# Attention and two FFN blocks on one core: the values product in high and low parts

## What is computed

```python
# attention: q, k, v are (4, 8, 576, 64), s is (4, 8, 576)
scores = scale * np.matmul(q, k.transpose(0, 1, 3, 2))
cum = np.cumsum(np.maximum(s, 0.0), axis=-1)
bias = -(cum[:, :, :, None] - cum[:, :, None, :])
scores = np.where(causal, -1000000000.0, scores + np.minimum(bias, 0.0))
attn = np.exp(scores - np.max(scores, axis=-1, keepdims=True))
attn = attn / (np.sum(attn, axis=-1, keepdims=True) + 1e-09)
x = np.matmul(attn, v)                    # heads side by side: (4, 576, 512)
# first FFN: x @ w_in (512 x 1024), relu h, 3-tap convolution c along the sequence,
x = (h * sigmoid(c)) @ w_out              # 1024 x 512
# second FFN: low-rank mixing along the sequence, then
u = x + (x^T @ U @ V)^T
out = u + relu(u @ w_ch1) @ w_ch2         # 512 x 2048, 2048 x 512
```

## Time and profile before

| | us |
|---|---|
| median of 3 runs | 1060.52 (1055.34 to 1065.8) |
| profiled execution, its own time | 1059.91 |
| its span, first to last instruction | 1058.1 |
| busy: PE / DVE / ACT / POOL | 947.3 / 506.0 / 348.7 / 170.4 |

### The profile page before, as it was taken

The page is one execution under the profiler, slowest core; times in us unless marked ns, Lnnn a source line. Parts: engine busy times, 40 slices in busy tenths (PEclk is TensorE's granted clock), DMA queues, the critical chain, the costliest instruction groups (busy, mean ns, idle before and its releaser), DMA issues.

```text
span 1058.1 us, 16893 instructions
## 1 busy us (share of the span) xinstructions
PE 947.3 (90%) x6395; PEld 881.2 (83%) x6395; DVE 506.0 (48%) x735; ACT 348.7 (33%) x662; POOL 170.4 (16%) x110
## 2 busy tenths in 40 slices
PE   3888887979999997988999999897999999789998
PEld 2766777869999987977899898796989999669998
DVE  4478884474344367165425247447334437332121
ACT  2445453443335144243323215334322314232020
POOL 2222164311333023000000003201000003100000
PEclk9899998998999999987999989899899999889999
DMA  4575554635665753342444544343255374223441
GB/s 96 137 206 159 132 152 146 210 85 170 223 197 175 261 170 114 126 119 79 126 154 159 182 159 144 119 131 98 90 160 173 123 222 167 90 107 120 162 164 79
DMA packets 72352, 155.69 MB, mean 147 GB/s; under 512 B 30356, under 2 KB 48788, under 8 KB 59992
## 3 DMA queue, kind: packets, MB, share of 16 engines
q1 hardware_dynamic: 72280, 154.66, 46.9%
HBM read 114.57 MB, written 30.03 MB: 137 GB/s over the span
## 4 chain that ended last, share of the span: by engine, by line
PE 64%; DVE 16%; issue 10%; POOL 3%; ACT 3%; DMA 2%; SPq 1%; POOLq 0%; DVEq 0%; ACTq 0%
PE psum L968 16%; PE psum L970 15%; PE psum L969 15%; PE psum L945 6%; POOL ybuf L502 3%; PE psum L891 3%; DVE sums L726 3%; DVE neg_max L713 2%; DVE work L763 2%; PE psum L922 2%; PE psum L924 2%; PE psum L905 1%; DVE max_split L717 1%; DVE qhl L702 1%; DVE work L760 1%
## 5 line engine op out<-in xcount | busy, mean ns | idle before, releaser
L968 PE MATMUL psum<-ybuf,ring 128*128 128x288 f32 x768 | 239.4, 312 | 28.4 <-POOL ybuf L502 20.5
L969 PE MATMUL psum<-ybuf,ring 128*128 128x288 f32 x768 | 232.0, 302 | 0.0
L970 PE MATMUL psum<-ybuf,ring 128*128 128x288 f32 x768 | 231.8, 302 | 0.0
L968 PEld LDWEIGHTS psum<-ybuf,ring 128*128 128x128 f32 x768 | 150.3, 196 | 33.3 <-POOL ybuf L502 25.5
L968 PE MATMUL psum<-uu_hl,ring 128*128 128x288 f32 x512 | 160.6, 314 | 13.4 <-DVE work L785 8.7
L713 DVE TENSOR_REDUCE neg_max<-psum 128x1 f32<-128x512 f32 (+4 forms) x165 | 83.4, 539 | 156.6 <-PE psum L896 150.0
L970 PE MATMUL psum<-uu_hl,ring 128*128 128x288 f32 x512 | 156.2, 305 | 0.0
L969 PE MATMUL psum<-uu_hl,ring 128*128 128x288 f32 x512 | 156.1, 305 | 0.0
L969 PEld LDWEIGHTS psum<-ybuf,ring 128*128 128x128 f32 x768 | 150.3, 196 | 0.8 <-issue 0.2
L970 PEld LDWEIGHTS psum<-ybuf,ring 128*128 128x128 f32 x768 | 149.8, 195 | 0.0
L493 POOL TENSOR_TENSOR klc<-kq_raw,khh 64x576 fp32r<-64x576 f32 x34 | 51.3, 1508 | 514.0 <-ACT khh L549 514.0
(11 more groups left out here) (89 smaller groups left out, 1479.9 us busy)
## 6 DMA issues: line engine op xcount, KB each, us to landing
ring<-w_scratch SPq DMA_DIRECT2D x72, 1024.0 KB, 4.8
w_scratch<-ring SPq DMA_DIRECT2D x24, 1024.0 KB, 6.0
...
```

The source lines that it names most:

```text
L968: pe.matmul(o, hi, m_hi, start=start, stop=False)
L969: pe.matmul(o, hi, m_lo, start=False, stop=False)
L970: return pe.matmul(o, lo, m_hi, start=False, stop=stop)
```

## The change

The values product becomes three fp32r products as well. For that the exponentials must exist in a high and a low part. ScalarE writes each chunk twice from PSUM: rounded to fp32r (`probs_hl[0]`) and in fp32 (`probs`); VectorE subtracts (`probs_low`, into `probs_hl[1]`). The buffers for them hold two chunks in place of four. The values are loaded to one buffer `v_raw`, rounded by ScalarE (`values_high`) and subtracted by VectorE (`values_low`), a head ahead. A PSUM bank of scores is free after both exponentials; a values product waits for the high exponentials and for the subtraction; SyncE's load of values waits for `values_low` of the head before.

```diff
-        va = [sb(f"va{i}", [P, NT, P], F32) for i in range(2)]
-        probs = sb("probs", [P, NC, BANK], F32)
+
+        v_raw = sb("v_raw", [P, NT, D], F32)
+        va_hi = [sb(f"va_hi{i}", [P, NT, P], F32R) for i in range(2)]
+        va_lo = [sb(f"va_lo{i}", [P, NT, P], F32R) for i in range(2)]
+        probs = sb("probs", [P, 2, BANK], F32)
+        probs_hl = [sb(f"probs_hl{i}", [P, 2, BANK], F32R) for i in range(2)]
...
-        exps = Count(sem("exps"), NC, 1)
+        exps = Count(sem("exps"), 2 * NC, 1)
+        p_low = Count(sem("p_low"), NC, 1)
...
                 def load_v(a, h):
-                    n, i, c0 = a * H + h, h % 2, D * (h % 2)
-                    mm_pv.wait(sp, n - 2)
+                    v_low.wait(sp, a * H + h - 1)
                     of = v[source(a, h)]
-                    sp.dma_start(va[i][:, 0:NT - 1, c0:c0 + D],
-                                 of[0:(NT - 1) * P, :].rearrange("(t p) d -> p t d", p=P)).then_inc(v_in[i].sem, 16)
-                    sp.dma_start(va[i][P - D:P, NT - 1, c0:c0 + D], of[(NT - 1) * P:S, :]).then_inc(v_in[i].sem, 16)
+                    sp.dma_start(v_raw[:, 0:NT - 1, :],
+                                 of[0:(NT - 1) * P, :].rearrange("(t p) d -> p t d", p=P)).then_inc(v_in.sem, 16)
+                    sp.dma_start(v_raw[P - D:P, NT - 1, :], of[(NT - 1) * P:S, :]).then_inc(v_in.sem, 16)
...
                 def exponentials(a, h, c):
-                    n = a * H + h
+                    n, x, w = a * H + h, c % 2, WIDTH[c]
                     mm_s.wait(act, n, c + 1)
-                    mm_pv.wait(act, n - 1, c + 1)
-                    act.activation(probs[:, c, 0:WIDTH[c]], psum[:, c % 2, 0:WIDTH[c]], ACT.Exp).then_inc(exps.sem, 1)
+                    mm_pv.wait(act, n, c - 1) if c >= 2 else mm_pv.wait(act, n - 1, c + 3)
+                    act.activation(probs_hl[0][:, x, 0:w], psum[:, x, 0:w], ACT.Exp).then_inc(exps.sem, 1)
+                    p_low.wait(act, n, c - 1) if c >= 2 else p_low.wait(act, n - 1, c + 3)
+                    act.activation(probs[:, x, 0:w], psum[:, x, 0:w], ACT.Exp).then_inc(exps.sem, 1)
+
+                def values_high(a, h):
+                    n, i, c0 = a * H + h, h % 2, D * (h % 2)
+                    v_in.wait(act, n)
+                    mm_pv.wait(act, n - 2)
+                    act.activation(va_hi[i][:, :, c0:c0 + D], v_raw[:, :, :], ACT.Copy).then_inc(v_high.sem, 1)
...
+                    if g == 3:
+                        values_high(a, h + 1)
...
                 prepare(0, 1)
+                values_high(0, 0)
                 max_to_row(0, 0)
...
+                def probs_low(a, h, c):
+                    n, x, w = a * H + h, c % 2, WIDTH[c]
+                    exps.wait(dve, n, 2 * c + 2)
+                    mm_pv.wait(dve, n, c - 1) if c >= 2 else mm_pv.wait(dve, n - 1, c + 3)
+                    dve.tensor_tensor(probs_hl[1][:, x, 0:w], probs[:, x, 0:w], probs_hl[0][:, x, 0:w].bitcast(F32),
+                                      ALU.subtract).then_inc(p_low.sem, 1)
+
+                def values_low(a, h):
+                    n, i, c0 = a * H + h, h % 2, D * (h % 2)
+                    v_high.wait(dve, n)
+                    dve.tensor_tensor(va_lo[i][:, :, c0:c0 + D], v_raw[:, :, :], va_hi[i][:, :, c0:c0 + D].bitcast(F32),
+                                      ALU.subtract).then_inc(v_low.sem, 1)
...
+                    if g == 0:
+                        probs_low(a, h, 0)
                     if g <= 2:
                         maxima(a, h + 1, g)
+                        probs_low(a, h, g + 1)
+                    if g == 4:
+                        values_low(a, h + 1)
...
                 for r in range(len(ROUNDS)):
                     maxima(0, 0, r)
+                values_low(0, 0)
                 query_low(0, 1)
...
-                    exps.wait(pe, n, c - 1) if c >= 2 else exps.wait(pe, n - 1, NC - 1 + c)
+                    exps.wait(pe, n, 2 * (c - 1)) if c >= 2 else exps.wait(pe, n - 1, 2 * (NC - 1 + c))
...
                 def values(a, h, c):
 
                     n, i = a * H + h, h % 2
-                    exps.wait(pe, n, c + 1)
+                    exps.wait(pe, n, 2 * c + 1)
+                    p_low.wait(pe, n, c + 1)
                     if c == 0:
-                        v_in[i].wait(pe, a * NPAIR + h // 2)
+                        v_low.wait(pe, n)
                         evict.wait(pe, n - 1)
                     at = WIDTH[c]
                     for t, i0, i1 in reversed(CHUNKS[c]):
                         lo, w = tile_rows(t)[0], i1 - i0
                         at -= w
                         first = (c, t) in ((0, 1), (3, 0))
-                        mm = pe.matmul(psf[:, O0 + i0:O0 + i1], va[i][lo:P, t, :], probs[lo:P, c, at:at + w],
-                                       start=first, stop=True, skip_group_check=True)
+                        o, p_hi, p_lo = psf[:, O0 + i0:O0 + i1], *(p[lo:P, c % 2, at:at + w] for p in probs_hl)
+                        pe.matmul(o, va_hi[i][lo:P, t, :], p_hi, start=first, stop=False, skip_group_check=True)
+                        pe.matmul(o, va_hi[i][lo:P, t, :], p_lo, start=False, stop=False, skip_group_check=True)
+                        mm = pe.matmul(o, va_lo[i][lo:P, t, :], p_hi, start=False, stop=True, skip_group_check=True)
                     mm.then_inc(mm_pv.sem, 1)
```

16 lines of the change are left out of this document (10 added, 6 removed).

## The result

The changed kernel takes **1128.45 us** (median of 4 runs, 1123.44 to 1130.06) against 1063.16 us: a ratio of 1.060, 95% interval 1.053 to 1.068. The forecast was 1095, its range ended at 1122. The profiled execution took 1123.44 us with a span of 1121.7; in the run shown ahead of the prediction the span was 1058.1, so 63.6 us are to be found.

What follows compares the result with a forecast made beforehand. TensorE was busy 90% of the span, so the price lay in attention chains without FFN cover. Terms 14 + 3 + 2 + 6 + 10.5 + 2 - 2 = 35.5 on 1059.91 gave 1095 us, range 1070 to 1122.

Steps and rivals of the forecast that it cites:

- the TensorE saving: Values products on TensorE: 0.07 to 0.27 us saved a head, counted only where TensorE is the bound; taken as -2.
- the heavier rival: VectorE/GpSimd holds on the path in 24 heads (+14, to 1108) plus lower TensorE clock (5 to 7): 1106 to 1130; chance 0.16.
- Entry: Entry of the second batch: x's low part for the first up product stands behind two more subtractions and a pair: +2.
- convolution: Up product with the convolution, once a batch: VectorE has 5.25 of 32 us free, gets 2.8 more: +6 (0 to 12).
- turn and mix: Ten light steps, two heads a batch: exponential pairs and subtractions delay the mix's add and turning steps: +10.5 (2 to 20).
- step-2 bursts: Step 2 of a head in the second FFN: VectorE has reductions, hold, subtractions, `query_low` ahead of FFN work: +2 (0 to 8).
- Attention alone: First batch's eight heads, without FFN cover: five heads 1.2 us later, three 2.7 later: +14 (6 to 20).
- the start: Head 1's values load waits for `values_low` of head 0, making the loads queued behind it 3.0 late: +3 (0 to 4).
- later loads: Values loads after the start wait for VectorE too, but four weight blocks lie ahead: nothing, or 1 us a batch if uncovered.
- 2.7 behind a normalised pair: Heads 3, 5 and 7 of the first batch: chunk 0's subtraction stands behind the normalisation, 2.7 us late each.
- Not slower: Rival: TensorE is the bound, the first batch too, so only the saving is left, 8.6 us at most: 1051; chance 0.07.
- lighter: Rival: every chain beside the FFN is hidden, only the start and first batch pay: 1070 to 1082; chance 0.17.

Runs made afterwards that it cites:

- b1: Changed kernel with more products that feed nothing before a head's first values product, 40 in heads 3, 5, 7 and 8 in others, first batch only: 1126.68 us.
- c1: The kernel before with none of its products that feed nothing: 1065.83 us, ratio 1.009.
- a3: Changed kernel with the exponentials' subtraction written to an unread buffer, TensorE not waiting for it, their low part zero: 1114.51 us, ratio 1.051.
- a2: Changed kernel with each exponential still written twice but no subtraction of exponentials, their low part zero; values still split: 1083.63 us, ratio 1.025.
- k5: Changed kernel with one exponential, no subtraction of exponentials or values, low parts zero; ScalarE's copy of values stays: 1073.73 us, four runs from 1060.23 to 1077.62.
- h4: Changed kernel with one exponential, no subtraction of exponentials (low part zero), and two buffers for the values as loaded: 1079.89 us, ratio 1.022.
- k6: Changed kernel with ScalarE's copy of the values moved behind the row of maxima, ahead of the head's eviction: 1133.89 us, ratio 1.070.
- b2: Changed kernel with the second half of each pair's normalisation moved behind the next head's first subtractions: 1129.09 us, ratio 1.068.
- d1: Changed kernel with two buffers for the values as loaded, so SyncE's load waits for the subtraction two heads back: 1121.58 us, ratio 1.059.
- h3: The kernel before with three fp32r products for each fp32 values product, identity matrix in place of the values: 1067.92 us, ratio 1.009.
- k4: The kernel before with four fp32r products for each values piece, identity matrix in place of the values: 1083.26 us, ratio 1.024.

## Why the prediction was wrong

**The sum has no term for TensorE's clock.** This is the step that failed. It priced waits and took every TensorE duration from the trace at full speed, with "the TensorE saving" of 2 on top; in the profile TensorE's own busy time grew by 37.6 us. The clock stood only in the heavier rival, as 5 to 7 us of the first batch. The profiled execution is 28 us over the 1095 of the sum. Of that, 21.1 lie beside the FFN (39.6 where 18.5 were priced, the saving taken off) and 8.2 in the first batch (25.2 where 17 were); the rest of the kernel is 1.2 shorter. Beside the FFN the 19.9 us of longer busy time had no term, and they are nearly all of the 21.1. That this is the clock is inferred, from the busy time and clock by stage: no run changes the clock alone beside the FFN.

A second estimate comes from repeated runs of one unchanged kernel. Over 56 runs of the kernel before, granted clocks of 0.933 to 0.959 go with 1067.1 to 1050.9 us, by a straight line 6.0 us for each 0.01. By that line, drawn on beyond its runs to 0.900, the 0.047 between the profiled executions are 28 us. It can't be the share of the clock in every stage: in the first batch b1 gave 2.4 us for 37 us at the lower level, while c1, with the old chains, gave 8.1 for 24. And a run with longer waits has a lower clock too, so the line may hold some of their time.

**Beside the FFN** the sum of the waits was right and its terms only in part, which is partly luck. Entry, convolution, turn and mix, and step-2 bursts made 2 + 6 + 10.5 + 2 = 20.5, and TensorE's idle time in batches 2 to 4 grew by 19.7. Read by periods from one turn of the maxima to the next, over the three batches:

| heads of a batch | beside them | priced | longer | idle longer |
|---|---|---|---|---|
| 0 | end of the FFN before, entry | 2 | 11.4 | 3.4 |
| 1 | up product with the convolution | 6 | 6.0 | 5.2 |
| 2 | down product | 0 | 0.0 | 0.1 |
| 3, 4 | most of turn and mix | 10.5 | 14.6 | 5.3 |
| 5 to 7 | second FFN | 2 | 7.6 | 5.7 |

The convolution's term was right. The idle time of turn and mix is half of its price, that of the second FFN is more than its own. At the entry of the second batch (head 8) nothing came as idle time: the period is 22.2 us in place of 16.8, at a clock of 0.68 in place of 1.00. a3 against a2 shows that the length of VectorE's subtractions brings nearly all of it, idle and busy, 35 us. ScalarE's pairs did not: the waits for its evictions (`hid`) are 12.4 us in a2, and 17.5 only with the subtractions.

**Attention alone** was 14, and 3 for the start, and is 25.2. The parts, by the first-batch column: products 1.7, copy and load of the values 8.4, their subtraction 2.7, the second exponential 1.5, the exponentials' subtraction 3.4 aside and 7.5 more with TensorE's wait. The last two, 10.9, are what the 14 was for. These are differences of single profiles, good to a microsecond or two. The term that was missing is the values' path, whose later loads were priced "at nothing": in k5 ScalarE waits 10.7 us for loads of values, three times, and in the changed kernel 5.5. All three are the loads that SyncE issues right behind a 1024 KB store and a 512 KB load of weights. The third in the changed kernel:

```profile
113.87 0.59 SPq L392 DMA_DIRECT2D w_scratch<-ring  x1
114.50 0.43 SPq L387 DMA_DIRECT2D stage<-in_w_out  x1
114.98 1.51 SPq L359 DMA_DIRECT2D v_raw<-in_v  x1
...
124.10 0.47 ACT L577 ACTIVATE va_hi<-v_raw 128x320 fp32r<-128x320 f32 x1 [4.26 <-DMA v_raw<-in_v]
```

In the first batch such loads land up to 7.5 us after their issue, where the median is 2.4. The kernel before issues them in the same order and they take up to 7.8, but nothing waits for them: there the values are wanted at the head's own first product, now at step 3 of the head before. A second buffer (h4) and the order on ScalarE (k6) leave that queue as it is, and gave no time back; no run moved the loads ahead of the weights, so how much that would give is open. The predicted 2.7 behind a normalised pair came as waits for the subtraction, four of up to 3.4 us, and b2 moved them for no gain in the whole.

**The start** went as worked out. SyncE's issues and `prepare` of head 2, beside the earlier trace rows:

```profile
20.91 0.40 SPq L359 DMA_DIRECT2D v_raw<-in_v  x1
...
22.06 0.51 SPq L368 DMA_DIRECT2D khc<-khh  x1
...
36.32 0.68 ACT L557 ACTIVATE khh<-kq_raw 128x576 fp32r<-128x576 f32 x1 [4.86 <-DMA kq_raw<-in_kq_t]
...
38.85 0.60 PE L960 MATMUL psum<-qhl,khh 128*128 128x320 f32 x1 [4.39 <-ACT qm L563]
```

22.0 and 36 were named; 22.06 and 36.32 are there. d1, without SyncE's wait, has a first batch 2.8 us shorter, so the price of 3 stands too.

**TensorE's saving** is right as a length and wrong as a price. A piece at full clock, beside the earlier trace rows:

```profile
113.69 0.38 PE L985 MATMUL psum<-probs_hl,va_hi 128*128 128x320 f32 x1 [1.51 <-DVE probs_hl L745]
...
113.91 0.30 PE L986 MATMUL psum<-probs_hl,va_hi 128*128 128x320 f32 x1
...
114.05 0.31 PE L987 MATMUL psum<-probs_hl,va_lo 128*128 128x320 f32 x1
```

The second and the third take 0.15 each. Where TensorE is the bound a head is 0.2 us shorter, within the 0.07 to 0.27 that were worked out. Over the whole kernel the form alone cost 10 us (h3), at a lower clock, and k4 shows that a fourth product raises the clock a little and doesn't pay either.

**The rivals.** Not slower and lighter are out. Heavier named its two causes, holds and clock; the clock was there, and the holds were small: GpSimd's busy time rose by 2.4 us, and holds of the new subtractions account for some 10 us of VectorE's (99.1 against 89), while its other operations took 8 less than before (497.9 against 506.0). Its 1108 by holds alone had no ground; its 1106 to 1130 holds the measured time, with other sizes for the two causes.
